# Second products of the 512-token blocks by seven block products, P1 copied between PSUM banks, queues reordered

## The reference

```python
def _moe_ref(x, domain_probs, w1, w2):          # 4 experts, w1 512x1024, w2 1024x512
    p = domain_probs / (domain_probs.sum(-1, keepdims=True) + 1e-09)
    out = 0
    for e in range(E):
        h = np.maximum(x @ w1[e], 0.0)
        out += p[:, e:e + 1] * (h @ w2[e])
    return out

def _moe2_ref(x, w_in, w_out):                  # 512x2048 and 2048x512
    h = x @ w_in
    return (h * np.cos(h)) @ w_out
```

## Time and profile before

| | us |
|---|---|
| median of 3 runs | 807.11 (806.55 to 807.96) |
| span of the profiled execution | 805.0 |
| attention, until the first product of the experts' stage | 44.7 |
| experts' stage | 44.7 to 535.0 |
| one quarter of it | 30.92 |
| MLP stage and end | 535.0 to 805.0 |
| PE, DVE, ACT, POOL busy | 797.7, 586.9, 297.5, 226.3 |

### The profile page before, as it was taken

The page is one execution under the profiler, slowest core; times in us unless marked ns, Lnnn a source line. Parts: engine busy times, 40 slices in busy tenths (PEclk is TensorE's granted clock), DMA queues, the critical chain, the costliest instruction groups (busy, mean ns, idle before and its releaser), DMA issues.

```text
span 805.0 us, 11348 instructions
## 1 busy us (share of the span) xinstructions
PE 797.7 (99%) x4372; PEld 675.1 (84%) x4372; DVE 586.9 (73%) x962; ACT 297.5 (37%) x564; POOL 226.3 (28%) x229
## 2 busy tenths in 40 slices
PE   8999999999999999999999999999999999999998
PEld 7888888888888888888888888888888888888886
DVE  6997866866866866757767668677787777777766
ACT  5853222221322322322322322256544545455442
POOL 3885433333343334334324333241000000000000
PEclk9999999999999999999999999999999999999999
DMA  9932111111100120101101111001111111111004
GB/s 326 372 118 66 40 27 39 49 57 40 40 26 27 53 66 27 50 18 39 40 27 40 30 37 40 27 27 26 39 28 39 27 27 40 39 28 27 0 1 156
DMA packets 19864, 44.81 MB, mean 56 GB/s; under 512 B 2344, under 2 KB 2392, under 8 KB 19812
## 3 DMA queue, kind: packets, MB, share of 16 engines
q1 hardware_dynamic: 19812, 44.10, 17.2%
HBM read 40.93 MB, written 3.17 MB: 55 GB/s over the span
## 4 chain that ended last, share of the span: by engine, by line
PE 95%; DMA 3%; DVE 1%; issue 0%; SPq 0%; DVEq 0%
PE ps L1053 33%; PE ps L1034 28%; PE ps L1134 16%; PE ps L1115 16%; DMA att<-att_in 3%; PE ps L1000 1%; PE ps L956 1%; PE ps L987 0%; DVE temps L807 0%; PE ps L970 0%; DVE temps L800 0%; SPq L291 0%; DVE y L903 0%; DVE temps L819 0%; DVE temps L839 0%
## 5 line engine op out<-in xcount | busy, mean ns | idle before, releaser
L458 POOL TENSOR_TENSOR h_lo<-temps,h_hi 128x512 fp32r<-128x512 f32 (+1 forms) x128 | 136.1, 1070 | 291.5 <-ACT h_hi L575 291.5
L788 DVE TENSOR_TENSOR y<-ps,y 128x512 f32<-128x512 f32 x180 | 121.8, 688 | 63.4 <-PE ps L1053 63.4
L575 ACT ACTIVATE h_hi<-temps 128x512 fp32r<-128x512 f32 (+1 forms) x128 | 67.3, 526 | 242.3 <-DVE temps L807 242.3
L1034 PE MATMUL ps<-x_hi,w_hi 128*128 128x512 f32 (+1 forms) x448 | 150.6, 336 | 0.5 <-DVE temps L800 0.5
L1034 PE MATMUL ps<-x_hi,w_lo 128*128 128x512 f32 (+1 forms) x448 | 150.5, 336 | 0.0
L1034 PE MATMUL ps<-x_lo,w_hi 128*128 128x512 f32 (+1 forms) x448 | 150.5, 336 | 0.0
L1053 PE MATMUL ps<-h_hi,w_hi 128*128 128x512 f32 x384 | 149.8, 390 | 0.0
L1053 PE MATMUL ps<-h_lo,w_hi 128*128 128x512 f32 x384 | 149.8, 390 | 0.0
L1053 PE MATMUL ps<-h_hi,w_lo 128*128 128x512 f32 x384 | 149.4, 389 | 0.0
L1034 PEld LDWEIGHTS ps<-x_hi,w_hi 128*128 128x128 f32 x448 | 84.9, 190 | 10.9 <-DVE temps L800 0.7
L1034 PEld LDWEIGHTS ps<-x_lo,w_hi 128*128 128x128 f32 x448 | 84.9, 190 | 9.9
(11 more groups left out here) (83 smaller groups left out, 1113.8 us busy)
## 6 DMA issues: line engine op xcount, KB each, us to landing
w_raw<-w_in SPq DMA_DIRECT2D x96, 256.0 KB, 2.7
att<-att_in SPq DMA_DIRECT2D x24, 512.0 KB, 7.2
temps<-p_scr SPq DMA_DIRECT2D x4, 768.0 KB, 5.3
out<-y SPq DMA_DIRECT2D x12, 256.0 KB, 2.0
att<-dp_in SPq DMA_DIRECT2D x1, 24.0 KB
p_scr<-att SPq DMA_DIRECT2D x1, 24.0 KB
lam<-lam_in SPq DMA_DIRECT2D x1, 6.0 KB, 1.6
```

Of the source, the lines that this page charges most:

```text
L458: pool.tensor_tensor(hs_lo[side][:, f, at], ring(s, i), f32(hs_hi[side][:, f, at]), ALU.subtract).then_inc(s_hlo, 1)
L575: act.activation(hs_hi[s % SIDES][:, f, at], ring(s, i), ACT.Copy).then_inc(s_hhi, 1)
L788: dve.tensor_tensor(at, from_bank, at, ALU.add).then_inc(s_y, 1)
L1034: mm = pe.matmul(ps[:, bank, 0:CTS[side]], ww[q % 2][:, of], xx[side][:, 2 * x + k, :], start=(opens and k == 0 and n == 0), stop=(k == 1 ...
```

## The change

- The second products of side 0 become a 2 by 2 block product as well: its two blocks of 512 tokens and the two halves of the quarter's 256 hidden rows, against the two halves of the 512 output columns. Seven products M1 to M7 of two units each (`m_unit`, three 512-wide matmuls) take the place of eight units of six. They accumulate in PSUM over one another (M1, M5, M6, M7 in banks 3 and 4; M3, then M2 and M4 in banks 5 and 6), and VectorE adds the running sum to a different block of `y` after each (`m_add`). Side 1 keeps its four ordinary units (`u_unit`, `u_add`).
- For that VectorE makes four sums of `h` in a quarter (`t_sum`, T1 to T4, 512 wide), which ScalarE and GpSimd split, and GpSimd makes four sums of `w2` (`w2_sums`), which become one more piece of weights (`w2_piece(q, 2)`, 1024 wide).
- Of the first products' assembly some moves into PSUM: ScalarE copies P1 from bank X to bank A (`copy_first`), P2 accumulates on that copy, P6, P7 and P4 accumulate on X. ScalarE also keeps P5 and P1+P6 in SBUF (`keep_fifth`, `keep_sixth`). VectorE's five sums become two (`sum_second`, whose result is written to PSUM, and `sum_third`), and three of the four weighted results read PSUM. One extra matmul into bank A is issued ahead of the stage.
- All queues are rewritten; side 0's M2, M4 and side 1's units of a quarter are computed in the next one. After the last quarter they stand alone ahead of the MLP stage. There is one probability buffer in place of two; two blocks of `y` are put together at the end of the stage (`combine`, four VectorE operations); the MLP stage takes the blocks in the order 1, 0, 2, and `LAG` is 5.

The diff, cut (removed lines other than two are left out):

```diff
--- before.py
+++ after.py
-FOLLOW = (((), (), (), (0,), (1,), (2,), (3,)), ((), (), (), (), (0, 1, 2, 3), (), (4, 5, 6, 7)))
...
+X, A, E = range(3)
+PRODUCTS = ((0, 0, X, True), (4, 4, X, False), (3, 3, E, True), (1, 1, A, False), (5, 5, X, False),
+            (2, 6, X, False), (6, 2, E, False))
+ORDER = (P1, P5, P6, P2, P3, P7, P4)
...
+M1, M5, M3, M6, M7, M2, M4 = range(7)
+SUM_1, SUM_2, SUM_3, SUM_4 = range(4)
+M_OPENS = (True, False, True, False, False, True, False)
+M_BANK = (3, 3, 5, 3, 3, 5, 5)
+M_FIRST = (True, True, True, False, True, False, False)
+U_BANK = (7, 3, 4, 7)
...
-LAG = 4
+LAG = 5
...
+            def w2_sums(q):
+                a11, a21 = w_raw[:, 2, 0:FF2], w_raw[:, 2, FF2:512]
+                a12, a22 = w_raw[:, 3, 0:FF2], w_raw[:, 3, FF2:512]
+                pool.wait_ge(s_raw[2], 16 * (q + 1))
+                pool.wait_ge(s_raw[3], 16 * (q + 1))
...
+                pool.tensor_tensor(w_sum[:, SUM_2, :], w_sum[:, SUM_1, :], a11, ALU.subtract).then_inc(s_wsum, 1)
+                pool.wait_ge(s_wsum, 8 * q + 7)
+                pool.tensor_tensor(w_sum[:, SUM_4, :], a12, w_sum[:, SUM_2, :], ALU.subtract).then_inc(s_wsum, 1)
...
+            for q in range(QUARTERS):
+                s = SIDES * q
+                more = q + 1 < QUARTERS
+                if q:
+                    t_low_of(q - 1, T4)
+                if q:
+                    w2_sums(q)
+                b_low(s, C11)
+                if more and q:
...
+                t_low_of(q, T2)
+                t_low_of(q, T3)
+                if q == 0:
+                    w_sums_part(1, 0)
+                    w_sums_part(1, 1)
+                    w_sums_part(1, 2)
+                b_low(s, C21)
+                if more:
+                    w_sums_part(q + 1, 3)
                 for i in range(4):
...
+                    side_low(s + 1, i)
+            t_low_of(QUARTERS - 1, T4)
+            for d in range(KT):
+                x2_low(0, d)
             for d in range(KT):
                 x2_low(2, d)
 
...
+            def copy_first(s):
+                width = CTS[s % SIDES]
+                act.wait_ge(s_prod, product_count(s, P1))
+                act.activation(ps[:, A, 0:width], ps[:, X, 0:width], ACT.Copy).then_inc(s_copy, 1)
...
+            def keep_sixth(s):
+                width = CTS[s % SIDES]
+                act.wait_ge(s_prod, product_count(s, P6))
+                act.activation(u2[:, 0:width], ps[:, X, 0:width], ACT.Copy).then_inc(s_u2, 1)
...
+            for q in range(QUARTERS):
+                s, last = SIDES * q, q == QUARTERS - 1
+                copy_first(s)
+                if q:
+                    w1_piece(q + 1, 0)
+                    keep_fifth(s)
+                    w1_piece(q + 1, 1)
+                    w2_piece(q, 2)
+                    keep_sixth(s)
+                    b_high(s, C11)
...
+                    keep_fifth(s)
+                    keep_sixth(s)
+                    b_high(s, C11)
+                    w2_piece(0, 2)
+                if q:
+                    w2_piece(q + 1, 0)
+                t_high_of(q, T1)
+                b_high(s, C21)
+                b_high(s, C22)
+                s += 1
+                copy_first(s)
...
+                t_high_of(q, T3)
+                if q == 0:
                     w1_piece(1, 0)
                     w1_piece(1, 1)
...
+            def m_add(q, j, only=None):
+                for t in range(2) if only is None else (only,):
+                    at, bank = m_rows(j, t), ps[:, M_BANK[j] + t, :]
+                    dve.wait_ge(s_m, m_count(q, j, t))
+                    if q and j in (M1, M5):
+                        dve.wait_ge(s_ym, y_count(q - 1, (M2, M4)[(M1, M5).index(j)], t))
+                    if j == M6:
+                        dve.wait_ge(s_ym, y_count(q, M3, t))
+                    if q == 0 and M_FIRST[j]:
+                        dve.tensor_copy(at, bank).then_inc(s_ym, 1)
+                    else:
+                        dve.tensor_tensor(at, bank, at, ALU.add).then_inc(s_ym, 1)
...
+            def sum_third(s):
+                width = CTS[s % SIDES]
+                dve.wait_ge(s_prod, product_count(s, P7))
+                dve.wait_ge(s_p5, s + 1)
+                if s >= 1:
+                    dve.wait_ge(s_hlo, h_low_count(s - 1, C21 if s % SIDES == 0 else C22))
+                dve.tensor_tensor(raw(s, C22), ps[:, X, 0:width], p5[:, 0:width], ALU.add).then_inc(s_c22, 1)
...
+                if i in (T2, T4):
+                    dve.wait_ge(s_t, 4 * q + (1, 1, 1, 2)[i])
+                one, two = ((b12, b11), (b22, raw_t(T1)), (b22, b12), (raw_t(T2), b21))[i]
+                dve.tensor_tensor(raw_t(i), one, two, ALU.subtract).then_inc(s_t, 1)
...
+            for q in range(QUARTERS):
+                s, last = SIDES * q, q == QUARTERS - 1
+                if q == 0:
                     x_sums(BLOCKS - 1)
                     x_lows(BLOCKS - 1)
...
+                else:
+                    m_add(q - 1, M2)
+                    u_add(q - 1, 0)
...
+                    w1_piece(q + 1, 1)
+                    w2_piece(q, 2)
+                else:
+                    w2_sum(SUM_1)
+                    w2_sum(SUM_3)
+                    w2_sum(SUM_2)
+                sum_second(s)
+                if q:
+                    u_add(q - 1, 2)
+                second_of(s)
+                sum_third(s)
+                if q == 0:
+                    w2_sum(SUM_4)
+                t_sum(q, T1)
+                third_of(s)
+                fourth_of(s)
+                if q == 0:
+                    dve.wait_ge(s_wlo, FIRST_PIECES)
+                    w2_piece(0, 2)
+                m_add(q, M1)
+                t_sum(q, T2)
+                if q:
+                    m_add(q - 1, M4)
+                t_sum(q, T3)
+                m_add(q, M5)
+                m_add(q, M3)
+                if last:
+                    u_add(q - 1, 3)
+                s += 1
+                sum_second(s)
+                first_of(s)
+                m_add(q, M6)
+                sum_third(s)
+                second_of(s)
+                third_of(s)
+                t_sum(q, T4)
+                fourth_of(s)
+                if q == 0:
                     w1_piece(1, 0)
                     w1_piece(1, 1)
...
+                m_add(q, M7, 0)
+                if q and not last:
+                    u_add(q - 1, 3)
+                if not last:
+                    w1_piece(q + 1, 2)
+                m_add(q, M7, 1)
+                if not last:
+                    w2_piece(q + 1, 0)
                     w2_piece(q + 1, 1)
...
+            def m_unit(q, j, t):
+                if t == 0:
+                    pe.wait_ge(s_hlo, low_count(q, j))
+                    pe.wait_ge(s_wlo, wlo_count(q, W2_2 if j in (M5, M3, M6, M7) else W2_1))
+                if j == M1 and q:
+                    pe.wait_ge(s_yu, KT * (q - 1) + 2 + t)
+                elif j in (M5, M6, M7):
+                    pe.wait_ge(s_ym, y_count(q, (M1, M5, M6)[(M5, M6, M7).index(j)], t))
+                elif j == M3 and q:
+                    pe.wait_ge(s_ym, y_count(q - 1, M4, t))
+                elif j in (M2, M4):
+                    pe.wait_ge(s_ym, y_count(q, (M3, M2)[(M2, M4).index(j)], t))
+                hi, lo = m_weights(q, j, t)
+                n = b_slot(q, j)
+                for m, (ww, hh) in enumerate(((hi, h_hi), (hi, h_lo), (lo, h_hi))):
+                    mm = pe.matmul(ps[:, M_BANK[j] + t, :], ww, hh[:, n, :], start=(M_OPENS[j] and m == 0),
+                                   stop=(m == 2), skip_group_check=True)
+                mm.then_inc(s_m, 1)
...
+            def second_products_ahead(q, i):
+                if i == P1:
+                    m_units(q, M2)
+                elif i == P5:
+                    u_unit(q, 0)
+                elif i == P6:
+                    u_unit(q, 1)
+                elif i == P3:
+                    u_unit(q, 2)
+                elif i == P7:
+                    m_units(q, M4)
+                elif i == P4:
+                    u_unit(q, 3)
+            def second_products_beside(q, i):
+                if i == P1:
+                    m_units(q, M1)
+                elif i == P6:
+                    m_units(q, M5)
+                elif i == P2:
+                    m_units(q, M3)
+                elif i == P7:
+                    m_units(q, M6)
+                elif i == P4:
+                    m_units(q, M7)
+            pe.matmul(ps[:, A, 0:CT], w1_hi0[:, 0:P], xs_hi[0][:, 0, :], start=True, stop=True)
...
+                    if i == P3:
+                        pe.wait_ge(s_p5, s + 1)
...
                     if i == P7:
...
+                        pe.wait_ge(s_u2, s + 1)
                     if i == P4:
...
+            last = QUARTERS - 1
+            m_units(last, M2)
+            u_unit(last, 0)
+            u_unit(last, 1)
+            m_units(last, M4)
```

(80 more changed lines are left out.)

591 lines of the change are left out of this document (311 added, 280 removed).

## The result

The changed kernel takes 792.3 us (median of 4 runs, 790.99 to 794.14), the kernel before 806.94 us beside it. The ratio is 0.982, with a 95% interval of 0.981 to 0.983. The forecast was 792.7 us. The sum came out right, its terms did not: the quarters from the second on lost 1.1 us where 4.8 were forecast, and the first quarter and the end lost 3 us more than forecast. That the two errors nearly cancel is luck.

What follows compares the result with a forecast made beforehand. PE was taken to bound the kernel, busy 797.7 of 805.0 us. -21.8 + 0.2 + 4.8 + 2.0 + 0.4 = -14.4 gave a span of 790.6, or 792.7 us as median; 8 in 10 range 786.8 to 803.

Steps and rivals of the forecast that it cites:

- PE's work: Second products: 66 matmuls for 72 a quarter, 1.36 us less in each of 16, -21.8 us; one extra matmul +0.2.
- Steady stalls: Ahead of M7: if T2 comes second to GpSimd's low of C22, PE waits 0.5; 0.3 a quarter taken, +4.8 us.
- my table: Hand layout of a quarter's queues with PE running through; 1.3 us of VectorE waits fit in before M7.
- The places with 0.4 to spare: Steady quarter: P4 behind `sum_third` and side 1's P1 behind `fourth_of` each have 0.4 us spare.
- no steady stall: Rival: VectorE wins the ties or finds other gaps in the quarters; 786.5 to 788.0 us, chance 0.24.
- shared path worse than my table: Rival: P5, P4 and M7 each late once, 0.7 to 1.3 us a quarter; 798 to 805.5 us, chance 0.16.
- Meetings for SBUF: VectorE operations with two SBUF inputs and GpSimd's block each other: VectorE waits 1.3 to 5.2 us a quarter.
- First quarter: P4 waits 0.9 to 1.5 us, M5 0.5 to 1, minus today's 0.5: +2.0 us (1 to 3).
- End: Units left behind the last quarter, ahead of the MLP stage: +0.4 us (0 to 1.5), the MLP stage itself 0.
- ScalarE, DMAs, `LAG`: ScalarE's extra copies and splits (13.3 us busy a quarter), DMA waits and `LAG` 5 in the MLP stage: 0.
- The sum: Terms total -14.4 us on the 805.0 span: 790.6; with the runs' 2.1 offset, 792.7 us.
- The rival in which VectorE is the bound: Slower: VectorE's waits exceed 4.2 us a quarter; at 5.2 the quarter is 31.9, total 825 us, chance 0.07.

Runs made afterwards that it cites:

- a_six_more: Changed kernel with P2's six side 0 matmuls issued twice from the second quarter on: 811.3 us.
- a_four_more: Changed kernel with four unneeded 512-wide VectorE reads of PSUM a quarter, two ahead of each of M5's adds: 809.72 us, ratio 1.0039.
- a_t2_late: Changed kernel with VectorE's T2 moved behind the first of M4's two adds: 791.23 us.
- v_first_end: Changed kernel with four VectorE queue moves, three in the first quarter, and both lows of the MLP's first `w2` at step 0: 793.24 us.
- v_second: Changed kernel with VectorE's first-quarter queue reordered (M1's adds earlier, T4 later) and the MLP's `w2` lows at steps 0 and 1: 791.54 us.
- a_fourteen_less: Changed kernel without the third matmul of each unit of M1 to M7, 14 matmuls fewer a quarter: 760.32 us.
- a_again: Changed kernel run once more, unchanged: 791.45 us, ratio 0.982.
- a_t2_early: Changed kernel with VectorE's T2 moved between M1's two adds: 793.35 us.
- v_third: v_second with two of GpSimd's sums of the next `w1` moved ahead of the low of T2 in the first quarter: 790.37 us, ratio 0.9805.
- a_pool_light: Changed kernel with GpSimd's four sums of `w2` made for 16 of 256 columns from the second quarter on: 792.08 us.

## Why the prediction was right in its sum and wrong in its terms

- **PE's work** (-21.8, +0.2): right. The trace has 672 + 384 = 1056 second-product matmuls, still 0.227 apart, and 6 matmuls are worth 1.36 us a quarter, as a_six_more shows. The period by count was 29.56 and is 29.62: five units of each quarter begin behind 256-wide matmuls and take 1.39 instead of 1.36. That is 0.06 net a quarter, 0.8 in all.
- **Steady stalls** (+4.8): wrong; PE waits in no quarter from the second on (the 0.3 us of the second is the restart behind the wait for its P1). The step that failed is "If not, T2 loses 1.1, T3 then meets T2's low and loses 0.6: PE waits 0.5", out of which I took 0.3 a quarter. The slack in that stretch was right, 1.3 us by my table and 1.3 to 1.6 by a_four_more. The delay set against it was not: I had 1.1 + 0.6 = 1.7 us, and it is 0 in the changed kernel (T2 and T3 take 0.68 each in every steady quarter) and 0.6 in a_t2_late, where T2 loses 0.6 and T3 nothing, since the low of T2 comes too late to meet it. Both lie below the slack, and PE waits for nothing. A case in which T2 loses 1.1 was never run. The places with 0.4 to spare (P4, side 1's P1) held in every steady quarter. The rival "no steady stall" had this part right, and that of a shared path worse than my table, with P5, P4 and M7 each late once a quarter, did not come about.
- **Meetings for SBUF**: the price lay in my range, the target was wrong. I expected T sums "well over 0.68"; they average 0.689. The meetings fall on weights: the low of `w2`'s sums 2.32 us instead of 1.2 in every quarter, as the table had it ("+1.1 us; that idle and the one ahead of P7 absorb it"), and the other two pieces of `w2` 1.18 and 1.22 instead of 0.68. With 0.1 to 0.4 for the sums of `w1` that is about 2.3 us a quarter, between my bounds of 1.3 and 5.2. The averages by line and shape (busy us, mean ns):

```profile
L1056 DVE TENSOR_TENSOR temps<-temps 128x512 f32<-128x512 f32 x64 | 44.0, 689 | 0.0
...
L917 DVE TENSOR_TENSOR w2s_lo<-w_sum,w2s_hi 128x1024 fp32r<-128x1024 f32 x16 | 37.1, 2318 | 0.0
```

VectorE's busy time, 26.27, is within the forecast of 25 to 27; GpSimd's, 20.1, is above 18 to 19, by waits inside its rows (its lows average 1475 to 1529 ns against 1362).
- **First quarter** (+2.0, range 1 to 3): mis-sized; 3.8. By the distances of starts P4's wait, forecast at 0.9 to 1.5, costs 1.2; M5's, forecast at 0.5 to 1, costs 1.4, since the low of `w2`'s sums takes 2.33 us and not 1.2, and M1's adds, for which M5 waits too, stand behind it. Two waits weren't in the sum: side 1's P1 (1.0) behind the fourth sum of `w2` (1.92 us where one beside no GpSimd operation takes 0.42), and the second quarter's P1 (0.8). I had checked those two places for the steady quarter alone, while VectorE has four more sums in the first. Together they are 4.4 us, and 0.4 more lies in small pieces. Of these 4.8 us 1.0 stood in the first quarter of before too, where I had deducted the 0.5 of its bracket. Each bracket costs 0.2 to 0.35 us more than it says. VectorE's timeline there:

```profile
51.33 0.42 DVE L1075 TENSOR_TENSOR w_sum<-w_sum,w_raw 128x256 f32<-128x256 f32 x1
...
53.60 1.92 DVE L1075 TENSOR_TENSOR w_sum<-w_raw,w_sum 128x256 f32<-128x256 f32 x1
...
57.25 2.33 DVE L917 TENSOR_TENSOR w2s_lo<-w_sum,w2s_hi 128x1024 fp32r<-128x1024 f32 x1
```

- **End** (+0.4, 0 to 1.5): mis-sized; 1.6. It is 0.8 for the last low of side 1 at 516.93 and 0.7 for the low of `w2` at the first `down2` (539.42), which an earlier low doesn't win back: in v_first_end and v_second PE waits there for a low of `h`. In every other quarter a first product P1 stands between the last M unit and the unit that needs this low; behind the last quarter there is none. I had put the MLP stage's share at 0.
- **ScalarE, DMAs, `LAG`** (0): right. ScalarE's copy from PSUM to PSUM takes 584 ns, the copies to SBUF 579 to 597. Nobody waits for it. It is busy 12.3 us a quarter where I had 13.3.
- **The sum** came out by luck. The steady quarters were 3.7 us better than forecast, the first quarter and the end 3.0 worse, and the stage began 0.7 earlier, for which there was no term. So the span is 789.2 where 790.6 was forecast. The medians, 792.3 and 792.7, lie closer because the profiled execution is the fastest of the four.
- **The rival in which VectorE is the bound** wasn't far off in kind: 2.4 us more of work a quarter, 2.7 by its rows, make PE wait for it in every quarter (a_four_more), and less work on PE does so too (a_fourteen_less). Its price of entry, 4.2 us of waits a quarter, was too high: the slack that counts is that of the stretch with a deadline, 1.3 to 1.6 us, and not that of the whole quarter.

What stays open: why the changed kernel's executions spread from 790.99 to 794.14 us in one run and by 0.5 us in a_again, why a_t2_early's median is 1.9 us above a_again's when its trace explains 1.1, and how the start of the experts' stage (43.5 to 45.1 us among the runs) comes to vary.

## What to carry to other kernels

Read slack per stretch between two hand-overs and set the expected delays against it; only what is left over reaches the engine that bounds the kernel. Where a delay comes from two engines meeting, lay out the second engine's queue as well before counting it: here two meetings were charged at 1.7 us, and the traces have one of 0.6 or none. A schedule that is periodic in the middle has a first and a last period in which a neighbour's work is missing: lay those out by hand too, for each queue; here they lost 5.4 us and the 14 quarters between them 1.1. A wait that goes when one queue is reordered can come back through the next engine's queue (v_first_end, v_second); look for that engine's idle time and fill it in the same edit (v_third).

## What the runs showed of the hardware

- An idle time of PE in brackets is short of its cost by 0.2 to 0.35 us (0.87 for 1.15 in a_four_more), and idle times of 0.08 to 0.17 us have no bracket at all: in a_fourteen_less PE lost 0.95 us a quarter with none shown. Distances between starts show them.
- Operations of VectorE with both inputs in SBUF can take over four times their own length when they meet GpSimd's: 1.92 us for a sum of 0.4. Two waits of that kind follow one another where both engines are queued up; in v_third the sums T2 and T3 take 2.92 us together beside GpSimd's sums of 1.19 (0.74 alone).
- Relief of this path moved busy time only: VectorE 0.5 us and GpSimd 2.1 us less in a quarter (a_pool_light), with no effect on a time that PE sets.
